# Two heads' rotation moved into the attention's tail, and score tiles placed between output steps

## The reference, cut to what matters

```python
def _attn_ref(q, k, v):                       # each (4, 8, 576, 64), float32
    q_rot, k_rot = rotate(q), rotate(k)       # x1*cos - x2*sin, x1*sin + x2*cos
    scores = np.matmul(q_rot, k_rot.transpose(0, 1, 3, 2)) / np.sqrt(D)
    scores = scores - np.max(scores, axis=-1, keepdims=True)
    attn = np.exp(scores)
    attn = attn / (np.sum(attn, axis=-1, keepdims=True) + 1e-09)
    return np.matmul(attn, v)

def _moe_ref(x, w_in, conv_w, w_out):         # x (4, 576, 512), d_ff 1024
    h = np.maximum(x @ w_in, 0.0)
    # conv_out: three taps of conv_w along the sequence, per channel of h
    gate = 1.0 / (1.0 + np.exp(-conv_out))
    return h * gate @ w_out
```

## Time and profile before

| what | value |
|---|---|
| median of 3 runs | 574.83 us (572.93 to 576.76) |
| the profiled execution | 577.52 us, its span 575.7 us |
| PE busy | 456.1 us (79%) |
| VectorE busy | 419.3 us (73%) |
| ScalarE busy | 280.5 us (49%) |
| GpSimd busy | 202.7 us (35%) |
| mean granted TensorE clock | 0.917 |

### The profile page before, as it was taken

One profiled execution on the slowest core, in us unless ns is written; L12 is line 12 of the kernel. 1 busy time (PEld: TensorE's weight loads), 2 busy tenths in 40 slices (PEclk: granted clock), 3 DMA queues, 4 the chain that ended last, 5 costly groups with the idle time before them and its releaser, 6 DMA issues.

```text
span 575.7 us, 17377 instructions
## 1 busy us (share of the span) xinstructions
PE 456.1 (79%) x6784; PEld 407.9 (71%) x6784; DVE 419.3 (73%) x796; ACT 280.5 (49%) x655; POOL 202.7 (35%) x277
## 2 busy tenths in 40 slices
PE   0045777859998699869998699869998698869996
PEld 0034656758998577659998477658998476659996
DVE  6978487727997987837997987836997979845441
ACT  1232555515766453525766453425666445425542
POOL 5312577522331254422331254421431244421221
PEclk9999979779999597979999597889999789889999
DMA  6888322025567011225567011224567102200011
GB/s 205 232 246 248 143 84 84 3 85 202 150 194 183 15 47 42 84 88 193 158 177 189 27 37 51 83 89 170 167 175 181 52 2 85 84 4 1 2 42 42
DMA packets 24368, 62.56 MB, mean 109 GB/s; under 512 B 3296, under 2 KB 7392, under 8 KB 21984
## 3 DMA queue, kind: packets, MB, share of 16 engines
q1 hardware_dynamic: 24288, 61.43, 34.3%
HBM read 42.55 MB, written 4.72 MB: 82 GB/s over the span
## 4 chain that ended last, share of the span: by engine, by line
PE 51%; DVE 18%; issue 12%; DMA 7%; POOL 4%; ACT 4%; SPq 2%; DVEq 0%; POOLq 0%; ACTq 0%
PE banks L366 15%; PE banks L338 6%; DVE neg_max L607 5%; PE banks L398 4%; PE banks L400 4%; PE banks L399 4%; PE banks L382 4%; PE banks L384 4%; PE banks L383 4%; DVE turned L632 3%; PE banks L339 3%; DVE conv L643 3%; DMA Q<-K 2%; DMA xs<-qk_swapped_dram 2%; DVE xs L592 2%
## 5 line engine op out<-in xcount | busy, mean ns | idle before, releaser
L472 ACT ACTIVATE P<-banks,neg_max 128x576 f32<-128x576 f32 x144 | 106.8, 742 | 134.3 <-DVE neg_max L607 133.2
L338 PE MATMUL banks<-K,Q 128*128 128x288 f32 x256 | 98.0, 393 | 76.1 <-ACT P L472 42.1
L607 DVE TENSOR_REDUCE neg_max<-banks 128x1 f32<-128x576 f32 x144 | 106.5, 742 | 42.0 <-PE banks L339 33.6
L338 PEld LDWEIGHTS banks<-K,Q 128*128 128x128 f32 x256 | 58.3, 228 | 104.6 <-ACT P L472 56.8
L761 POOL TENSOR_SCALAR P<-P,recip 128x576 f32<-128x576 f32 x124 | 91.9, 752 | 103.3 <-DVE recip L624 103.3
L366 PE MATMUL banks<-turned,V 32*64 32x128 f32 (+1 forms) x4608 | 109.9, 322 | 21.6 <-DVE turned L632 20.4
L765 POOL TENSOR_TENSOR u_lo<-u,u_hi 128x288 fp32r<-128x288 f32 x64 | 61.9, 968 | 173.8 <-ACT u_hi L505 173.8
L366 PEld LDWEIGHTS banks<-turned,V 32*64 32x64 f32 x4608 | 90.3, 146 | 33.9 <-issue 29.2
L632 DVE STREAM_TRANSPOSE turned<-P 128x576 f32<-128x576 f32 x144 | 109.0, 761 | 3.2 <-PE banks L366 3.1
L643 DVE SCALAR_TENSOR_TENSOR conv<-banks,taps,conv 128x288 f32<-128x288 f32 x128 | 65.8, 514 | 37.7 <-ACT conv L494 37.4
L339 PE MATMUL banks<-KL,Q 128*128 128x288 f32 x256 | 84.3, 340 | 0.0
(11 more groups left out here) (50 smaller groups left out, 620.2 us busy)
## 6 DMA issues: line engine op xcount, KB each, us to landing
V<-v_rows_dram SPq DMA_DIRECT2D x16, 1152.0 KB, 5.1
xc<-qk_dram SPq DMA_DIRECT2D x28, 288.0 KB, 2.9
xs<-qk_swapped_dram SPq DMA_DIRECT2D x28, 288.0 KB, 4.2
KL<-Q SPq DMA_DIRECT2D x32, 144.0 KB, 3.8
Q<-K SPq DMA_DIRECT2D x32, 144.0 KB, 3.6
K<-K SPq DMA_DIRECT2D x32, 144.0 KB, 3.0
y_dram<-y_sb SPq DMA_DIRECT2D x8, 576.0 KB, 3.3
wi_raw<-w_in_dram SPq DMA_DIRECT2D x1, 2048.0 KB, 8.0
```

What stands on the lines that cost most here:

```text
L338: nc.tensor.matmul(out, Q[:, h, qc], K[:, h, cols], start=True, stop=False)
L472: nc.scalar.activation(dst, src, ACT.Exp, bias=neg_max[:, c:c + 1], scale=1.0, accum_out=row_sum[:, c:c + 1]).then_inc(exps, 1)
L607: nc.vector.tensor_reduce(out=neg_max[:, c:c + 1], in_=banks[:, 2 * (t % 2):2 * (t % 2) + 2, 0:HALF], axis=AX.XY, op=ALU.max, negate=True) ...
```

## The change

Two of the eight heads of the next batch (`GAP` = 2) are rotated ahead of `x_low(b, 3)` on VectorE and ahead of `x_high(b, 3)` on ScalarE; the other six take the MLP's places of heads 0 to 5. SyncE loads the next batch's heads once the V product of pair 2 is done, and V behind the waits on the seventh and eighth head. TensorE puts score tiles 0 to 4 one by one behind output steps 11 to 15. ScalarE copies the second half of y behind the exponentials of four tiles, not of two. VectorE turns tiles 0 and 1 inside `first_maxima`, and waits for the output steps and the stored result at the turns of tiles 5 and 9, not ahead of the attention.

```diff
+    GAP = 2
@@ prepare (SyncE)
                     if not starting and j == 6:
                         store_y(b - 1, 0)
+                    if not starting and j == H - 1:
+                        load_v(b, 0)
+                    if not starting and j == H:
+                        values_read(b - 1, 3)
+                        load_v(b, 1)
@@ batch (SyncE)
                 values_read(b, 2)
-                load_v(b + 1, 0)
-                values_read(b, 3)
-                load_v(b + 1, 1)
                 prepare(b + 1)
                 store_y(b, 1)
@@ gated_mlp (TensorE)
-                    if not last and UNITS <= n < UNITS + 2:
-                        pe.wait_ge(gated, b * UNITS + (UNITS - 2 if n == UNITS else UNITS))
+                    if not last and n >= UNITS:
+                        if n < UNITS + 2:
+                            pe.wait_ge(gated, b * UNITS + (UNITS - 2 if n == UNITS else UNITS))
                         score(b + 1, *FIRST_TILES[n - UNITS])
                 if not last:
-                    for tile in FIRST_TILES[2:]:
+                    for tile in FIRST_TILES[LAG:]:
                         score(b + 1, *tile)
@@ gated_mlp (ScalarE)
-                    if not last and n % 2 == 1 and 3 <= n <= 2 * H + 1:
-                        rope_high(b + 1, n // 2 - 1)
+                    if not last and n % 2 == 1 and 3 <= n <= 2 * (H - GAP) + 1:
+                        rope_high(b + 1, GAP + n // 2 - 1)
                 if not last:
-                    for tile in FIRST_TILES[:2]:
+                    for tile in FIRST_TILES[:4]:
                         exp_tile(b + 1, *tile)
                 copy_y(b, 1)
                 if not last:
-                    for tile in FIRST_TILES[2:-1]:
+                    for tile in FIRST_TILES[4:-1]:
                         exp_tile(b + 1, *tile)
-                    act.wait_ge(y_stored, (2 * b + 2) * 16)
-                    act.wait_ge(rope_lo, (b + 1) * H + H)
@@ loop (ScalarE)
+                for j in range(GAP):
+                    rope_high(b + 1, j)
                 x_high(b, PAIRS - 1)
@@ turn (VectorE)
+                if not isinstance(b, int) and t == FULL + 1:
+                    dve.wait_ge(y_step, b * UNITS)
+                if not isinstance(b, int) and t == TILES:
+                    dve.wait_ge(y_stored, 2 * b * 16)
@@ attention, gated_mlp, first_maxima (VectorE)
-                turn(b, 0)
-                turn(b, 1)
...
-                    if not last and n % 2 == 1 and n // 2 < H:
-                        times_cos(b + 1, n // 2)
-                        times_sin(b + 1, n // 2)
+                    if not last and n % 2 == 1 and n // 2 < H - GAP:
+                        times_cos(b + 1, GAP + n // 2)
+                        times_sin(b + 1, GAP + n // 2)
...
-                    dve.wait_ge(y_step, b * UNITS + UNITS)
-                    dve.wait_ge(y_stored, (2 * b + 2) * 16)
...
                 normalise_group(b, 0)
+                turn(b, 0)
                 max_tile(b, 0, 4)
...
                 normalise_group(b, 1)
+                turn(b, 1)
                 max_tile(b, 0, 5)
@@ loop (VectorE)
+                for j in range(GAP):
+                    times_cos(b + 1, j)
+                    times_sin(b + 1, j)
+                    rope_add(b + 1, j)
+                for j in range(GAP):
+                    rope_low(b + 1, j)
                 x_low(b, PAIRS - 1)
@@ gated_mlp (GpSimd)
-                if not last:
-                    pool.wait_ge(y_step, b * UNITS + UNITS)
```

More of the change, by code:

```diff
@@ L683, in gated_mlp @@
                         tap(b, n, 2, tap1, tap2)
[L684 to L687, removed]
-                    if not last and n % 2 == 1 and n // 2 < H:
-                        times_cos(b + 1, n // 2)
-                        times_sin(b + 1, n // 2)
+                    if not last and n % 2 == 0 and 2 <= n <= 2 * (H - GAP):
+                        rope_add(b + 1, GAP + n // 2 - 1)
+                    if not last and n % 2 == 1 and 3 <= n <= 2 * (H - GAP) + 1:
+                        rope_low(b + 1, GAP + n // 2 - 1)
+                    if not last and n % 2 == 1 and n // 2 < H - GAP:
+                        times_cos(b + 1, GAP + n // 2)
+                        times_sin(b + 1, GAP + n // 2)
                     if not last and n == TAIL_STEP:
```

## The result

| | before | after |
|---|---|---|
| median of the runs (range) | 575.80 us (572.93 to 580.98, 4 runs) | 568.75 us (566.52 to 570.49, 4 runs) |
| the profiled execution, its span | 577.52 us, 575.7 us | 570.49 us, 568.6 us |

The recorded ratio is 0.9856, with a 95% interval of 0.9815 to 0.9898: 1.4% faster, where 1.25% was forecast. It isn't the quotient of the two medians above, which is 0.9878 (7.05 us, 1.2%); both lie in the interval. The sum was made against the profiled execution of before and gave 570.3 us for it; 570.49 us came. So near a hit is partly luck, since executions of one kernel range over 4 to 8 us. In the tables of the experiments medians and ranges are of all runs of a kernel, while the ratios leave out its few slow ones (three of `e1_rotation_alone`, one each of `e2_order_alone` and `e9_hole_filled`).

What follows compares the result with a forecast made beforehand. TensorE bounds the passage from MLP to attention until the last output step, then VectorE's list. Three passages at 2.7 us gained less 0.3 for the clock give 7.2 us, so 574.83 becomes 567.6 us, range 563 to 572.5.

Steps and rivals of the forecast that it cites:

- The bound and the mechanism: Passage from MLP to attention: VectorE's list pulled forward beside TensorE's output steps, 2.7 us a passage, 8.1 us in all.
- maximum 4 earlier: VectorE at the passage: maximum 4 starts at 445.2 instead of 447.24, 2.0 us.
- the transposes: VectorE between maximum 4 and maximum 6: tile 0's transpose moves ahead of maximum 4 into a gap, saving 0.68 us.
- the rebuilt order of TensorE: TensorE at the passage: score tiles between output steps, none waiting for exponentials; output step 15 ends at 444.0.
- rival C: No change: the attention's start isn't what is late, tiles 6 to 13 fall in with GpSimd or moves; 574 us, chance 0.07.
- a drain behind the table load: ScalarE: the skill's 1.38 us drain would make score 2 some 0.3 us late, the sum about 1 us smaller; not counted.
- The waits moved, SyncE's order, y's copy: Moved waits, stores and V loads on SyncE, and ScalarE's later copy of y (1.13 us) were all put at nothing.
- The clock given back: TensorE's clock returning later against the work, around the first V products: 0.3 us a passage lost, bounds -0.6 to +1.3.
- rival B: The clock takes half: V products run one more step at 0.50, 1.3 us a passage, 4 us back; 571 us, chance 0.17.
- E's hope: Better: the clock stays up as TensorE's holes shrink, tiles 6 to 13 cost less, 2 us a passage more; 562, chance 0.05.
- The rotation in the gap: VectorE ahead of `x_low`: at most 6.9 us of work, cover 1 to 2.4 us; cost 0, bounds 0 to 1 a batch.
- rival D: Slower: late loads in the gap starve TensorE, costing from 2.4 us delay, whole gain at 5.1; 581 at 7, chance 0.05.

Runs made afterwards that it cites:

- e1_rotation_alone: The changed kernel with two heads rotated in the gap and V's loads moved, but TensorE's and ScalarE's order and the transposes as before: 575.52 us, 0.998 of before.
- e2_order_alone: The changed kernel with all eight heads in the MLP's loop and loads as before, keeping the new orders and transposes: 577.12 us, 0.9997 of before.
- e9_hole_filled: The changed kernel with 16 extra unread matmuls ahead of each batch's last V product on TensorE: 570.39 us, 0.9869 of before.
- e4_turns_back: The changed kernel with the transposes of tiles 0 and 1 put back ahead of the maximum of tile 6: 571.24 us, 0.9903 of before.
- e7_delay_6: The changed kernel with six unread VectorE maxima (4.04 us) between the rotation in the gap and `x_low`: 578.04 us, 1.0009 of before.
- e8_filled: The changed kernel with extra unread matmuls behind score tiles 5 to 12 of batches 2 to 4: 567.24 us, 0.9833 of before.
- e6_unroll_dve: The changed kernel with only VectorE's loop over the batches written out: 571.03 us in its one execution.
- e10_both_filled: The changed kernel with extra unread matmuls both behind score tiles 5 to 12 and ahead of the last V product: 569.10 us, 0.9880 of before.

## Why the prediction was right, step by step

**The bound and the mechanism: right.** The gain at maximum 6 is 2.67 us in the mean of three passages (2.16, 2.72, 3.13), 2.7 was summed. Its two terms: maximum 4 earlier by 1.97 (2.0), the transposes 0.7 (0.70 in `e4_turns_back`). Counted from score tile 0, the rebuilt order of TensorE came as listed, to 0.2 us: score tiles and output steps without a wait from 431 to 441. No change (rival C) is out by the passage's marks, and `e1` and `e2` show that what the sum took from both parts can't be had from one. By the prediction's own figures a drain behind the table load would make score tile 2 late by 0.1 us (439.8 against 439.7) and not 0.3; it plays no part, as the rows have no room for one.

**The waits moved, SyncE's order, y's copy: right.** VectorE has no idle time ahead of a transpose between 445 and 462 (its idle there is ahead of maxima, for TensorE), and the copy starts at 183.74 without a wait and ends at 184.87, before maximum 4 (184.70 to 185.46) feeds exponential 4.

**The clock given back: the number by luck.** 1.0 us of 8.0 went, 0.3 a passage, as summed, but not where it was placed. Between maximum 6 and the first V product 0.2 us are lost in all three batches together. The rest is the balance of 1.8 us more at the last V product, a term that the prediction put at nothing, and of 0.8 us won elsewhere. The first and the second batch meet their V products at 1.37 and 1.40 us, the third at 2.31, so rival B's step at 1.2 GHz came once, not in every batch, and before had it in the same batch. E's hope, that the clock stays up by itself, didn't come (0.51 in the window above); `e8_filled` shows that it would have been worth 5.2 us up to the first V products. The period between passages came out at 127.8 us in the mean: the 127.3 of the prediction's list leaves its own 0.3 for the clock out.

**The rotation in the gap: right in its cost, wrong in its reasons.** In the change no row shows a cost: `x_high` starts 0.05 to 0.08 us behind the V product's end. `e4_turns_back`, with the same gap, shows 1.2 us in one batch, just over the bound of 1 us. And the cover was 0.2 and 0.8 us in batches 2 and 3, where 1 to 2.4 us were forecast. The step that failed is "head 1 is there at 383.4, when VectorE comes to it (381.2 and three instructions)": VectorE comes 2.5 to 3 us later, since the loop's way back (2.52 and 3.15 us) lay in front. In the third batch the 0.8 us were there only because the V product took 0.8 us longer than before. Issuing the four loads took 3.0 us (372.64 to 375.68), where 2 were put. And rival D's "it begins to cost from 2.4 us of delay" failed, whether its 2.4 us are the upper end of the cover or the early hidden matmuls: `e7_delay_6` shows every microsecond behind `x_low`'s idle paid. Loads at twice the median would land at 387.6, 3.8 us after VectorE comes to them, which is well over a cover of 1 to 2.4, and not "not much more". For more work on VectorE D's threshold was thus 0.2 us in the second batch, and 4 us of delay ate the whole gain (forecast: 5.1). For the loads, D's own mechanism, there was more room than seen: in batches 2 and 3 they land during the way back, as the start at 248.91 in `e6_unroll_dve` shows against 251.95 in the change.

## What to carry to other kernels

When two engines bound a passage in turn, price the edits together and apart: freeing VectorE's list and giving TensorE's tiles out earlier were worth 0.2% and 0.0% alone, neither to be told from nothing, and 1.4% together. Idle time at the head of a hardware loop's body isn't all free for work: subtract the loop's way back, which a wait of the same length hides. And count a chain's slack once: matmuls that already cover `x_high` and `x_low` cover nothing that is put ahead of them.

## What the hardware showed that was not expected

- The way back of a hardware loop took 2.5 to 3.2 us on VectorE in the change and 2.0 to 4.2 in the other kernels with the loop (idle called "issue", gone in the unrolled kernels). On TensorE 3.96 and 4.59 us of the same idle show in `e10_both_filled`, where the row of the change names only the semaphore that it then waits for; that this is the loop too is argued, not shown.
- Unrolling all five engines' loops changed the time by nothing that can be measured (0.9851 against 0.9856).
- Filling matmuls hold the granted clock at 1.00 where it was 0.51 and win 5.2 us by the marks, but the runs show only 0.2% in the middle, inside the intervals. In batches 2 and 3 the clock was down for most of the last V product instead (0.57 in the window of the third).
